# Pooled scores of the streamed attention pairs placed directly behind the local scores in TensorE's order

## The reference

```python
q_d = q.reshape(B, H, Sd, factor, D).mean(axis=3)   # k_d, v_d likewise; factor 4
out_up = np.repeat(sm_attn(q_d, k_d, v_d), factor, axis=2)
...
mask = np.abs(pos[:, None] - pos[None, :]) < factor
scores = np.where(mask, scale * np.matmul(q, k.transpose(0, 1, 3, 2)), -1000000000.0)
...                                                  # softmax of the rows, times v
return (out_up + out_local)

h = x @ w_in                                         # x: 2304 tokens x 512
x = (h * np.clip(h + 3.0, 0.0, 6.0) / 6.0) @ w_out
h = np.maximum(np.maximum(x @ w1, x @ w2), x @ w3)   # second layer
out = h @ w_out
```

## Time and profile before

| | us |
|---|---|
| median of 3 runs (lowest, highest) | 773.63 (773.39, 774.57) |
| the profiled execution | 774.09 |
| its span | 772.3 |
| TensorE busy | 756.3 |
| VectorE, ScalarE, GpSimd busy | 435.1, 285.7, 221.0 |
| granted TensorE clock, mean | 0.998 |

### The profile page before, as it was taken

The page is one execution under the profiler, slowest core; times in us unless marked ns, Lnnn a source line. Parts: engine busy times, 40 slices in busy tenths (PEclk is TensorE's granted clock), DMA queues, the critical chain, the costliest instruction groups (busy, mean ns, idle before and its releaser), DMA issues.

```text
span 772.3 us, 13368 instructions
## 1 busy us (share of the span) xinstructions
PE 756.3 (98%) x5254; PEld 670.6 (87%) x5254; DVE 435.1 (56%) x822; ACT 285.7 (37%) x623; POOL 221.0 (29%) x280
## 2 busy tenths in 40 slices
PE   7889999999999999999999999999999999999998
PEld 5667777878888788778999999999989999899996
DVE  5866676367556646653556756266771656535650
ACT  4845544343343334334444435222241221412211
POOL 7864866321122022201247650022200111011110
PEclk9999999999999999999999999999999999999999
DMA  9994633223302331301436886787014750137202
GB/s 182 190 235 101 157 64 65 48 70 64 64 18 47 84 83 21 61 18 56 177 115 260 306 330 215 255 344 257 30 41 130 279 192 1 56 123 279 103 2 81
DMA packets 123851, 100.48 MB, mean 130 GB/s; under 512 B 89996, under 2 KB 108428, under 8 KB 123788
## 3 DMA queue, kind: packets, MB, share of 16 engines
q1 hardware_dynamic: 121108, 98.75, 42.1%
q10 hardware_dynamic: 2680, 0.89, 0.6%
HBM read 73.66 MB, written 25.95 MB: 129 GB/s over the span
## 4 chain that ended last, share of the span: by engine, by line
PE 89%; DVE 4%; POOL 3%; ACT 1%; DMA 1%; issue 1%; SPq 1%; DVEq 0%; POOLq 0%
PE bank L885 28%; PE bank L886 27%; PE bank L887 27%; PE bank L1025 1%; PE bank L1002 1%; PE bank L991 1%; DMA k_nat_c<-in_k_dram 1%; PE bank L947 1%; PE bank L964 1%; PE bank L977 1%; POOL w L798 1%; POOL dp_a L790 1%; SPq L519 0%; ACT dp_a L1251 0%; ACT rg L1319 0%
## 5 line engine op out<-in xcount | busy, mean ns | idle before, releaser
L885 PE MATMUL bank<-xo,wt 128*128 128x384 f32 x378 | 126.3, 334 | 0.0
L887 PE MATMUL bank<-xo,wt 128*128 128x384 f32 x378 | 126.3, 334 | 0.0
L886 PE MATMUL bank<-xo,wt 128*128 128x384 f32 x378 | 126.3, 334 | 0.0
L1688 DVE SCALAR_TENSOR_TENSOR rg<-rg,bank 128x512 f32<-128x512 f32 (+1 forms) x80 | 50.5, 632 | 127.1 <-ACT rg L1319 126.8
L885 PE MATMUL bank<-xs,w 128*128 128x512 f32 (+1 forms) x320 | 120.9, 378 | 0.9 <-DVE xs L1656 0.9
L885 PE MATMUL bank<-gs,w 128*128 128x512 f32 (+1 forms) x320 | 120.4, 376 | 0.6 <-DVE y L1702 0.5
L887 PE MATMUL bank<-xs,w 128*128 128x512 f32 (+1 forms) x320 | 118.0, 369 | 0.0
L886 PE MATMUL bank<-xs,w 128*128 128x512 f32 (+1 forms) x320 | 117.9, 368 | 0.0
L886 PE MATMUL bank<-gs,w 128*128 128x512 f32 (+1 forms) x320 | 117.7, 368 | 0.0
L887 PE MATMUL bank<-gs,w 128*128 128x512 f32 (+1 forms) x320 | 117.6, 368 | 0.0
L1319 ACT ACTIVATE rg<-bank,half 128x512 f32<-128x512 f32 (+1 forms) x80 | 51.5, 644 | 150.1 <-PE bank L887 150.1
(11 more groups left out here) (252 smaller groups left out, 1137.2 us busy)
## 6 DMA issues: line engine op xcount, KB each, us to landing
wt<-t_scratch SPq DMA_DIRECT2D x19, 1792.0 KB, 7.6
t_scratch<-ph SPq DMA_DIRECT2D x9, 896.0 KB, 3.6
t_scratch<-pl SPq DMA_DIRECT2D x9, 896.0 KB, 5.7
b_raw<-in_moe_w_dram SPq DMA_DIRECT2D x9, 512.0 KB, 4.0
xr<-x_scratch SPq DMA_DIRECT2D x3, 1536.0 KB, 10.0
out_dram<-o_sb SPq DMA_DIRECT2D x18, 256.0 KB, 2.0
w_raw<-in_moe_w_in_dram SPq DMA_DIRECT2D x16, 256.0 KB, 3.9
w_raw<-in_moe_w_out_dram SPq DMA_DIRECT2D x16, 256.0 KB, 4.9
```

Of the source, the lines that this page charges most:

```text
L885: mm(dst, w[0], m[0], start=start, stop=False, skip_group_check=True)
L886: mm(dst, w[0], m[1], start=False, stop=False, skip_group_check=True)
L887: return mm(dst, w[1], m[0], start=False, stop=stop, skip_group_check=True)
L1688: vec.scalar_tensor_tensor(out=gated(s), in0=gated(s), scalar=1.0, in1=hidden_bank(s)[:, 0:n], op0=ALU.min, op1=ALU.mult).then_inc(s_g, 1)
```

## The change

```diff
@@ -1031,7 +1031,6 @@
                 for n, i in at_slot(slot):
                     if i == STAGES[1]:
                         scores_local(n)
-                    if i == STAGES[2]:
                         scores_down(n)
                     if i == STAGES[3]:
                         turn_local(n)
```

## The result

The change made the kernel slower: 797.70 us median (796.30 to 797.91) against 773.59, ratio 1.031 (95% interval 1.029 to 1.032), 24.1 us more. The forecast was 790.6, or 17.0 us more. The measured time lies just inside the upper end of the range (798), and only part of the way there is the forecast's.

The account below looks back on a forecast made before the run. TensorE, busy 756.3 of 772.3 us, was taken to bound the kernel. Moved pairs 16.67 + 0.86 for the transposes' wait - 0.57 for y = 16.96 us, so 791.05 from the profiled 774.09, 790.6 as median; range 787 to 798.

Parts of the forecast that it names:

- the main term: TensorE at pairs 5 to 15: each loses new idle time less a saved passage, W - 0.96; sum 16.67 us.
- W: Time from start of local scores to start of pooled ones, set by VectorE's masking; forecast 2.33 to 2.87 us.
- the saved passage of 0.22: TensorE, each moved pair: one switch between small and large matmuls fewer, saving about 0.22 us.
- the waits for y: Output groups at pairs 8 and 12 wait for copies of the sums (L1702); both waits go, -0.57 us.
- three waits that react: Existing TensorE waits: pair 6's before pooled transposes +0.86 us, two for y -0.57 us, pair 4's 0.9 stays.
- the chain through GpSimd: Pair 6: GpSimd's product follows the hidden group behind the pooled scores; transposes lose 0.86 us of cover.
- The forecast's own place of reference: Pair 4, already in the new order: pooled scores start 2.25 us after local ones, with 1.45 us idle.
- the wait for dp_a: TensorE before the pooled transposes (L991) at pair 6, waiting for GpSimd: grows by 0.86 us, bounds 0 and 0.86.
- the clock: Rival: TensorE's clock also falls at the new gaps; one fall 792.4, three 795.9, eleven 809.9 us; chance 0.27.
- price of 1.75 a fall: TensorE's clock at half rate: a fall costs about half of 3.5 us, 1.75 us.
- its band for the gap: TensorE idle length at which the clock's fall is decided: somewhere between 1.45 and 2.01 us.
- the likeliest case: Idle time less saved passages plus reacting waits, without falls: 790.6 us, own range 787.5 to 793, chance 0.64.

Follow-up runs that it names:

- the two edits of that queue: Changed kernel with VectorE turning k and pooling q and k one slot earlier: 791.33 us; changed kernel with an extra mask copy delaying the masking: 811.91 us.
- The exchange on ScalarE: Changed kernel with ScalarE taking the gate's high half before the pooled exponentials, for pairs of even FIRST: 792.85 us.
- ScalarE's exchange in both kernels: Gate's high half before the pooled exponentials, in the kernel before: 773.37 us; in the changed kernel with 12 extra matmuls in the wait: 789.89 us.
- the filled kernel: Changed kernel with 12 extra matmuls between local and pooled scores of pairs 5 to 15: 794.87 us; also with the gate's high half first: 789.89 us.
- even-slot pairs alone: Only pairs 5 and 7 have pooled scores directly behind the local ones, all other pairs as in the kernel before: 777.65 us, ratio 1.005.
- gate first: Changed kernel with the gate's high half before the pooled exponentials on ScalarE, for pairs of even FIRST: 792.85 us.
- early k: Changed kernel with VectorE turning k and pooling q and k one slot earlier for pairs 5 to 15: 791.33 us.
- both together: Changed kernel with k turned and pooled one slot earlier on VectorE and the gate's high half first on ScalarE: 787.38 us, ratio 1.017.
- masking put off: Changed kernel with an extra VectorE copy of the mask into lp, which the masking waits for, for pairs 5 to 15: 811.91 us.

## Why the prediction was right and where it was wrong

**Right: the place and the main term.** The forecast read the wait from pair 4 and carried it to eleven pairs by the start of the masking. The measured W of pairs 5 to 15 are 2.46, 2.71, 2.46, 2.33, 2.73, 2.33, 2.33, 2.33, 2.86, 2.33, 2.33, none off by more than 0.01. The pairs that have nothing else on them, 5 and 7, lost 1.51 and 1.52 against 1.50 and 1.51, so the saved passage of 0.22 was right too. That the masking hangs on VectorE's queue is shown by the two edits of that queue.

**Right: the waits for y.** They went, and gave back 0.29 each.

**Wrong: the step "three waits that react".** It named the chain through GpSimd as the one that loses 0.86 us of cover, and looked for the others only among waits that existed. The same hidden group also feeds a shorter chain: relu, gate, high half behind the pooled exponentials on ScalarE, low half on VectorE, and the next but one output group waits for that. The timeline of VectorE in the kernel before, for pair 9, shows how near it was:

```profile
191.10 1.08 DVE L1695 TENSOR_TENSOR gs<-rg,gs 128x512 fp32r<-128x512 f32 x1 [0.95 <-ACT gs L1325]
```

It ended at 192.18, and the group that reads it started at 192.74. In the kernel after each of the nine waiting groups starts 0.06 us behind the end of the low half (231.66 and 231.72 at pair 10), so there were 0.50 us of room. The chain lost 0.86 of cover: at pair 10 the group starts 0.36 later than in a plain stream, its second matmul starts 0.34 behind the first instead of 0.23, and by the distances the whole is 0.49, at nine pairs 4.4 us. The exchange on ScalarE removes that.

The forecast's own place of reference had it. Pair 4 ran in the changed order all along, and this is TensorE and VectorE three groups behind its pooled scores in the kernel before:

```profile
63.27 0.39 PE L887 MATMUL bank<-xs,w 128*128 128x512 f32 x1
63.76 0.50 PE L885 MATMUL bank<-gs,w 128*128 128x512 f32 x1
64.09 0.39 PE L886 MATMUL bank<-gs,w 128*128 128x512 f32 x1
...
62.62 1.08 DVE L1695 TENSOR_TENSOR gs<-rg,gs 128x512 fp32r<-128x512 f32 x1 [0.95 <-ACT gs L1325]
```

The group starts 0.49 us behind the matmul ahead of it, where the stream has 0.23, and 0.06 behind the low half (63.70). The idle time in it is 0.10 us, and the list of waits had no row for it; only the starts show it.

**Mis-sized: the wait for dp_a**, 0.38 instead of 0.86. The gs wait stands ahead of it on TensorE and takes up the rest of the same delay: at pair 6 both together are 0.87. With ScalarE's exchange in both kernels, and so without a wait for gs, the wait at pair 6 is 0.32 in the kernel before and 1.20 in the filled kernel:

```profile
115.10 0.69 PE L991 MATMUL bank<-ident,dp_a 72*72 72x72 f32 x8 [0.32 <-POOL dp_a L790]
...
119.50 0.69 PE L991 MATMUL bank<-ident,dp_a 72*72 72x72 f32 x8 [1.20 <-POOL dp_a L790]
```

The first line is from the kernel before, the second from the filled one. That is 0.88 more, against the forecast's 0.86. So the lost cover was sized rightly; what was missing is that a second chain loses the same cover and shows first.

**Open by its own words, and it came: the clock.** It had the chance of 0.27; the forecast put the falls outside its sum. Two falls of 1.6 each are 3.2 us. The forecast's price of 1.75 a fall was nearly right, and so was its band for the gap, 1.45 to 2.01 us; that long matmuls stand around each gap, its argument against a fall, did not prevent one. The Trainium skill ("TensorE: Matmul & The Clock Gate", section "HAM oscillation — how this bites in real kernels") names as harmful a gap longer than any here. Read as a limit below which nothing happens, as the forecast tried it, that does not hold for this mix of matmuls: gaps of 1.65 us and more were followed by falls, though not each of them.

**Why it was still inside the range.** The forecast missed 7.1 us: 4.4 for gs, 3.2 for the clock, less 0.5 for dp_a. The range reached upward for falls of the clock alone, and more than half of what it reached for was used by the wait for gs. Without the falls the change would have been near 794.9, as in the filled kernel, outside the 787.5 to 793 of the likeliest case; with one fall more than the two it would have been beyond 798. That the time lies inside the range is partly luck: room left for one cause was taken up by another.

## What to carry to other kernels

When a step is moved out of the space between a producer and its user, list every chain that starts at that producer and read each one's room in microseconds, not only the ones that already wait: the cover that goes is the same for all. The gap itself then has a second price, its effect on the clock. If a wait on TensorE cannot be avoided, matmuls of no use inside it kept the clock here and cost nothing, since they ended before the wait did (W stayed 2.33). And if one place already runs in the new order, read its starts to the end of every chain, not only its first wait.

## What the runs showed of the hardware

**Falls of the clock by the length of the gap.** TensorE idle between 40 matmuls 64x64 and 8 of 64x144, in the middle of 128x512 groups; counted in the profiled executions of the changed kernel and of five experiments without filling (even-slot pairs alone, gate first, early k, both together, masking put off):

| idle gap, us | gaps | followed by a fall |
|---|---|---|
| 1.10 | 16 | 0 |
| 1.32 to 1.34 | 2 | 0 |
| 1.44 to 1.46 (pair 4) | 6 | 0 |
| 1.51 to 1.52 | 12 | 0 |
| 1.65 | 12 | 2 |
| 1.90 to 1.92 | 10 | 6 |
| 2.05 | 2 | 2 |
| 2.32 to 2.82 | 3 | 3 |

Equal gaps in one execution went both ways, so in this band the length of the gap alone does not decide; what else does was not found. The runs of such a kernel spread by as much as 5.5 us. Each fall that was priced cost 1.6 us, and the clock came back under the large matmuls.

**Two heads side by side.** The pooled matmuls of two heads, on rows 0 to 63 and 64 to 127 and into two banks, take 0.64 us for eight records, which start two by two; on the same rows and into one bank they start one by one, 0.12 us apart, and take 1.13. The experiment changed rows and bank together, so which of the two does it is not shown.
